# Attention and two FFNs on one core: all softmax sums by way of gathered rows, weights of V with 65 columns and full last key tiles, first head and first layer in another order

## The chip, the cores and the metric

The kernel runs on one core of one Trainium2 chip. The metric is the device time of one execution in microseconds (us). TensorE does the matrix products, VectorE (DVE) and ScalarE (ACT) the elementwise work, GpSimd (POOL) a few fills and the DMA issues of the sums, SyncE (SP) all other DMA issues.

## What is computed

Four batches (B = 4), eight heads (H = 8) of 576 positions (S) and head size 64 (D). First attention with a causal mask and a bias from running sums, then two FFNs:

```python
scores = q @ k^T / 8
cum = cumsum(max(s, 0));  bias = min(-(cum[query] - cum[key]), 0)
attn = exp(masked(scores + bias) - max);  attn /= sum(attn) + 1e-9
x = heads side by side of (attn @ v)                      # (B, 576, 512)

h = max(x @ w_in, 0)                                      # 512 -> 1024
c = three-tap convolution of h over the positions
x1 = (h * sigmoid(c)) @ w_out                             # 1024 -> 512

u = x1 + (V^T U^T applied over the positions of x1)       # rank 32
out = u + max(u @ w_ch1, 0) @ w_ch2                       # 512 -> 2048 -> 512
```

## The kernel before

Each tensor of the FFN is held transposed (channels on partitions, 576 positions in the free dimension, in halves of 288), split into a high and a low part, so that each product is three matmuls (function `three`).

**Attention** of one head runs in five steps, g = 0 to 4. The queries are 576 columns and the keys come in five tiles of 128 rows; the last one starts at 448, so that its first 64 rows repeat keys of tile 3, and only its last 64 are used. First the maximum of each query is found. `max_scores` makes scores with queries on partitions in three rounds (`ROUNDS`), `maxima` on VectorE reduces them, `max_transpose` turns the maxima into a row on TensorE and `max_to_row` on ScalarE writes it as row 96 of `qc`. This is done one head ahead. Then `scores` makes scores with keys on partitions in four chunks, `exponentials` takes exp of each on ScalarE, and `values` multiplies with V, chunk c in step g = c + 1; these are float32 matmuls, two instructions for each product. In the text a "visit" is one such call. The tile `va` held V in 64 of its 128 columns and ones in the other 64, in the order of the head's parity, so that the sums of the exponentials come out on 64 partitions beside the 64 of the result. `evict_head` copies both out of PSUM. The tile of the last keys was used from its row 64 on (`lo = tile_rows(t)[0]`).

Head h + 2 is prepared during head h: ScalarE writes `kb` and `qb` (rounded), VectorE their low parts (`key_low`, `query_low`). In batch 0 VectorE also copies the high parts (`highs`); from head 10 on ScalarE does that.

**Normalising.** For pairs 0 to 2 of a batch's four pairs of heads, one row of sums per head goes by `gather_sums` (DMA) onto 64 partitions of 9 numbers each, is inverted there (`invert_few`), stored (`store_few`), and read back broadcast to all partitions (`spread_few`, two DMAs); `normalise_few` multiplies. For pair 3 `evict_head` copied the 64 rows of sums, and `normalise` did two reciprocals of 128x288 and two products. Then `x_high` (ScalarE) and `x_low` (VectorE) split the pair, which is a fourth of the first layer's contraction; the pairs of a batch must all be there for its first item, `wi`.

**Order.** Each engine executes lists written out by hand. Batch 0's attention runs alone (`ATT_STEPS`, 40 steps). Then batch a's attention is run beside the FFN of batch a - 1, whose items (`wi`, `gated`, `wo`, `turn`, `rank`, `mix`, `up`, `down`, each for a half) `spread` deals to the steps by estimated costs; for a = 1 the first three steps stay empty. What is left after the last attention is the list `END`. An item's PSUM bank is reused two items later (in `END` four). `attention_step` is called before the items of a step and `then` behind them. VectorE runs its `then(a, h, g)`, and in batch 0 after it the low half of a block of weights at g = 2 of the heads in `WEIGHTS_HEADS`, and at `UV_AT` the splitting of U and V. All engines take their instructions in order.

```python
for (h, g), beside in zip(ATT_STEPS, PLAN[a]):
    attention_step(a, h, g)
    for item in beside:
        ffn_step(item)
    if then:
        then(a, h, g)
```

## Time and profile before

| | |
|---|---|
| median of 3 runs (lowest to highest) | 934.64 us (931.06 to 935.13) |
| the profiled execution's own time | 932.81 us |
| its span in the trace | 931.0 us |
| TensorE matmuls busy | 883.0 us (95%), 6184 instructions |
| VectorE busy | 482.5 us (52%), 992 |
| ScalarE busy | 373.2 us (40%), 709 |
| GpSimd busy | 40.4 us (4%), 83 |
| mean granted TensorE clock | 0.987 |

In the rows below "start us, us" are the start and the duration of the first to the last of the merged instructions; "[2.39 <-DVE x_hl L877]" says that the engine sat idle 2.39 us before it, until that instruction. Matmuls are pipelined: their durations overlap, so the pace is read from the distances of their starts. A float32 product with its high and low part counts as two instructions. PEclk is the granted clock as a share of 2.4 GHz.

### The profile page before, as it was taken

How to read it: one execution, taken by the hardware profiler on the slowest of the kernel's cores; microseconds unless marked ns; L12 is line 12 of the kernel's file. 1: busy time of each engine (PE TensorE's matmuls, PEld its weight loads, DVE VectorE, ACT ScalarE, POOL GpSimd, SP SyncE). 2: the span in 40 equal slices, each digit the busy share in tenths (PEclk: the TensorE clock that was granted, in tenths of full speed). 3: DMA queues.
4: the chain of work that ended last, by engine and by line, in shares of the span. 5: the costliest groups of instructions: out<-in, count | busy, mean ns of one | idle time of the engine just before them, and what ended most of it. 6: DMA issues, size and time to landing. Idle time of an engine off the chain costs nothing.

```text
span 931.0 us, 15627 instructions
## 1 busy us (share of the span) xinstructions
PE 883.0 (95%) x6184; PEld 833.6 (90%) x6184; DVE 482.5 (52%) x992; ACT 373.2 (40%) x709; POOL 40.4 (4%) x83
## 2 busy tenths in 40 slices
PE   3988898989999999999999999999999999999998
PEld 2766798969999999898999999988999999999998
DVE  6677796364447852645335872356324670442222
ACT  2656585464334644534323653344221441321110
POOL 3011000010000000000000000001000000000000
PEclk9989999999999999999999999999999999999999
DMA  6576455643764546546444433534343434454441
GB/s 169 125 193 177 126 168 182 232 125 99 242 219 147 171 139 181 202 113 198 153 152 156 168 148 126 167 123 143 116 149 136 180 138 161 157 187 169 150 180 51
DMA packets 63340, 147.04 MB, mean 158 GB/s; under 512 B 29482, under 2 KB 43818, under 8 KB 50980
## 3 DMA queue, kind: packets, MB, share of 16 engines
q1 hardware_dynamic: 60964, 142.40, 46.8%
q0 software_dynamic: 2304, 3.65, 1.5%
q8 instruction: 49, 0.80, 0.4%
q14 instruction: 23, 0.19, 0.1%
HBM read 115.87 MB, written 30.09 MB: 157 GB/s over the span
## 4 chain that ended last, share of the span: by engine, by line
PE 81%; DVE 10%; ACT 5%; issue 3%; DMA 1%; SPq 0%; POOL 0%; ACTq 0%; DVEq 0%
PE psum L1143 22%; PE psum L1145 21%; PE psum L1144 21%; PE psum L1124 8%; PE psum L1071 3%; PE psum L1103 2%; PE psum L1101 2%; DVE psum L849 2%; DVE kb L828 1%; PE psum L1108 1%; DVE qb L836 1%; DVE sums L869 1%; DVE work L914 1%; ACT qc L650 1%; ACT kb L635 1%
## 5 line engine op out<-in xcount | busy, mean ns | idle before, releaser
L1143 PE MATMUL psum<-uu_hl,ring 128*128 128x288 f32 x512 | 155.7, 304 | 7.4 <-DVE uu_hl L952 2.8
L1143 PE MATMUL psum<-r_hl,ring 128*128 128x288 f32 x512 | 154.4, 302 | 1.1 <-DVE u_acc L969 1.1
L1145 PE MATMUL psum<-uu_hl,ring 128*128 128x288 f32 x512 | 151.5, 296 | 0.0
L1144 PE MATMUL psum<-uu_hl,ring 128*128 128x288 f32 x512 | 151.4, 296 | 0.0
L1145 PE MATMUL psum<-r_hl,ring 128*128 128x288 f32 x512 | 151.2, 295 | 0.0
L1144 PE MATMUL psum<-r_hl,ring 128*128 128x288 f32 x512 | 151.1, 295 | 0.0
L1124 PE MATMUL psum<-probs,va 128*128 128x320 f32 (+4 forms) x448 | 124.1, 391 | 6.4 <-ACT probs L656 6.4
L957 DVE SCALAR_TENSOR_TENSOR r_hl<-psum,r_hl 128x288 fp32r<-128x288 f32 x128 | 58.4, 457 | 132.6 <-ACT r_hl L748 132.6
L748 ACT ACTIVATE r_hl<-psum 128x288 fp32r<-128x288 f32 x128 | 52.4, 410 | 181.3 <-PE psum L1145 181.2
L849 DVE CUSTOM_DVE_ANT_0 psum<-psum,key_late 128x512 f32<-128x512 f32 (+4 forms) x160 | 84.8, 564 | 60.3 <-PE psum L1071 59.8
L656 ACT ACTIVATE probs<-psum 128x320 f32<-128x320 f32 (+2 forms) x128 | 61.4, 501 | 115.2 <-PE psum L1108 86.8
L1143 PEld LDWEIGHTS psum<-uu_hl,ring 128*128 128x128 f32 x512 | 96.8, 189 | 11.2 <-DVE uu_hl L952 4.4
L1143 PEld LDWEIGHTS psum<-r_hl,ring 128*128 128x128 f32 x512 | 96.6, 189 | 3.7 <-DVE u_acc L969 1.8
L1144 PEld LDWEIGHTS psum<-uu_hl,ring 128*128 128x128 f32 x512 | 96.9, 189 | 0.3
L1144 PEld LDWEIGHTS psum<-r_hl,ring 128*128 128x128 f32 x512 | 96.6, 189 | 0.6
L1145 PEld LDWEIGHTS psum<-uu_hl,ring 128*128 128x128 f32 x512 | 96.7, 189 | 0.0
L1145 PEld LDWEIGHTS psum<-r_hl,ring 128*128 128x128 f32 x512 | 96.5, 188 | 0.0
L969 DVE TENSOR_TENSOR u_acc<-psum,u_acc 128x288 f32<-128x288 f32 x96 | 43.2, 456 | 102.2 <-PE psum L1145 102.2
L1124 PEld LDWEIGHTS psum<-probs,va 128*128 128x128 f32 (+1 forms) x448 | 75.9, 196 | 16.4 <-ACT probs L656 8.7
L1143 PE MATMUL psum<-x_hl,ring 128*128 128x288 f32 x256 | 79.3, 310 | 4.0 <-DVE x_hl L877 3.4
L1101 PE MATMUL psum<-qb,kb 128*128 128x320 f32 (+4 forms) x224 | 80.8, 378 | 2.1 <-ACT qc L650 1.2
L1143 PE MATMUL psum<-ybuf,ring 128*128 128x288 f32 x256 | 76.7, 300 | 0.0
(103 smaller groups left out, 1648.1 us busy)
## 6 DMA issues: line engine op xcount, KB each, us to landing
ring<-w_scratch SPq DMA_DIRECT2D x72, 1024.0 KB, 4.8
w_scratch<-ring SPq DMA_DIRECT2D x24, 1024.0 KB, 5.3
kq_raw<-in_kq_t SPq DMA_DIRECT2D x64, 288.0 KB, 5.2
stage<-in_w_ch SPq DMA_DIRECT2D x16, 512.0 KB, 5.2
out_t<-u_acc SPq DMA_DIRECT2D x16, 288.0 KB, 4.0
va<-in_v SPq DMA_DIRECT2D x32, 128.0 KB, 2.3
spread_out<-few_scratch POOLq DMA_DIRECT2D x24, 144.0 KB, 3.5
stage<-in_w_in SPq DMA_DIRECT2D x4, 512.0 KB, 7.5
```

Of the source, the lines that this page charges most:

```text
L656: act.activation(probs[:, c % 2, 0:WIDTH[c]], psum[:, c % 2, 0:WIDTH[c]], ACT.Exp).then_inc(exps.sem, 1)
L748: act.activation(r_hl[0][:, f, cols(half)], half_at("up", b, unit, f, half), ACT.Relu).then_inc(rh.sem, 1)
L849: dve.tensor_tensor_reduce(psf[:, at:at + width], psf[:, at:at + width], key_late[:, S - width:S], 1.0, LEAST, ALU.add, ALU.max, row_max[: ...
L957: dve.scalar_tensor_tensor(out=r_hl[1][:, f, cols(half)], in0=half_at("up", b, unit, f, half), scalar=0.0, in1=r_hl[0][:, f, cols(half)].b ...
L969: dve.tensor_tensor(u_acc[:, d, cols(half)], half_at("down", b, unit, d, half), so_far[:, d, cols(half)], ALU.add)\
L1071: mm = pe.matmul(psf[:, at + j:at + e], qc[i][0:CROWS, q0:q0 + P], kc[n % KCS][0:CROWS, j:e], start=bank not in started, stop=True, skip_g ...
L1101: pe.matmul(o, kb[i][:, k0:k0 + P], qb[i][:, i0:i1], start=(x == 0), stop=False, skip_group_check=True)
L1103: mm = pe.matmul(o, kc[n % KCS][:, k0:k0 + P], qc[i][:, i0:i1], start=False, stop=True, skip_group_check=True)
L1124: mm = pe.matmul(psf[:, O0 + i0:O0 + i1], va[i][lo:P, t, :], probs[lo:P, c % 2, at:at + w], start=first, stop=True, skip_group_check=True)
L1143: pe.matmul(o, hi, m_hi, start=start, stop=False)
L1144: pe.matmul(o, hi, m_lo, start=False, stop=False)
L1145: return pe.matmul(o, lo, m_hi, start=False, stop=stop)
```

## The change

- `va` holds V in columns 0 to 63 and ones in column 64 for both parities. `values` uses 65 columns as weights and writes partitions 0 to 64. The first 64 rows of the last key tile are zeroed once, and the product runs over all 128 rows. So does `rank` over its last tile.
- All four pairs are normalised by gathered sums. `normalise` is gone. Pair 3 is inverted and normalised in the next batch's head 0: at steps (0, 1) and (0, 4) beside batch 1, at (0, 0) and (0, 1) beside batches 2 and 3, and in `END` before items 2 and 5. A gather now waits for the copy of the sums alone.
- Beside batch 1 six steps stay empty of FFN items. Pair 2 of batch 0 is normalised at head 7, pairs 0 and 1 one step sooner within heads 4 and 6 (g = 2). The low parts of pairs 0 and 1 move from g = 0 to g = 2. Pairs 2 and 3 are split at steps (0, 0) and (1, 0) of batch 1.
- First head: VectorE does head 0's low parts and maxima before it copies head 1; the last round of scores has PSUM banks of its own, and needs no wait. For all other heads that round's wait is split by bank: what goes into the first bank waits for one reduction, the rest for three.
- GpSimd starts its fills for heads 1 and 2 after the running sums; TensorE waits for the last fill (`s_zero`) only before the first attention step.
- The fourth block of weights is prepared at head 5 for head 6, U and V are split at (3, 2) for (3, 4).

```diff
@@ -239,10 +238,14 @@
+        def max_at(n, r, t):
+            return MAX_AT[t][0] - 2 * BANK * (n == 0 and r == 2), MAX_AT[t][1]
         GROUPS = 5
-        WEIGHTS_HEADS = [1, 2, 4, 6]
-        UV_AT = (3, 4)
+        WEIGHTS_HEADS = [1, 2, 4, 5]
+        UV_AT = (3, 2)
@@ -326,10 +329,9 @@
                   for a in range(1, B)}
-        PLAN = {a: spread(BESIDE[a], len(ATT_STEPS) - 3 * (a == 1), 3 * (a == 1), a == 1) for a in BESIDE}
+        PLAN = {a: spread(BESIDE[a], len(ATT_STEPS) - 6 * (a == 1), 6 * (a == 1), a == 1) for a in BESIDE}
         END = order(B - 1, second(B - 2, UNITS // 2, UNITS)) + flat(second(B - 1, 0, UNITS))
-        END_NORMALISE = (0, 1)
-        END_SPLIT = 2
+        END_INVERT, END_NORMALISE, END_SPLIT = 2, 5, 6
@@ -411,7 +413,11 @@
         X_SPLIT = [{(5, 0): 0, (7, 0): 1}, {(3, 4): 0, (5, 4): 1, (7, 4): 2}]
-        X_SPLIT_LAST = [{}, {(0, 2): (NPAIR - 2, NPAIR - 1)}, {(0, 2): (NPAIR - 1,)}]
+        X_SPLIT_LAST = [{}, {(0, 0): (NPAIR - 2,), (1, 0): (NPAIR - 1,)}, {(0, 2): (NPAIR - 1,)}]
+        NORMALISE = [(4, 6, 7), (3, 5, 7)]
+        INVERT_LAST = [(0, 1), (0, 0)]
+        NORMALISE_LAST = [(0, 4), (0, 1)]
@@ -444,14 +450,14 @@
                 def load_v(a, h):
-                    n, i, c0 = a * H + h, h % 2, D * (h % 2)
+                    n, i = a * H + h, h % 2
                     if n >= B * H:
                         return
                     mm_pv.wait(sp, n - 2)
                     of = v[source(a, h)]
-                    sp.dma_start(va[i][:, 0:NT - 1, c0:c0 + D],
+                    sp.dma_start(va[i][:, 0:NT - 1, 0:D],
                                  of[0:(NT - 1) * P, :].rearrange("(t p) d -> p t d", p=P)).then_inc(v_in[i].sem, 16)
-                    sp.dma_start(va[i][P - D:P, NT - 1, c0:c0 + D], of[(NT - 1) * P:S, :]).then_inc(v_in[i].sem, 16)
+                    sp.dma_start(va[i][P - D:P, NT - 1, 0:D], of[(NT - 1) * P:S, :]).then_inc(v_in[i].sem, 16)
@@ -574,6 +580,8 @@
                 pool.wait_ge(s_mask, 6)
+                pool.wait_ge(s_scan, 1)
@@ -585,30 +593,35 @@
                 copied.wait(pool, 0)
                 for i in range(2):
-                    pool.memset(va[i][:, :, D * (1 - i):D * (1 - i) + D], 1.0)
+                    pool.memset(va[i][:, :, D:D + 1], 1.0).then_inc(s_va, 1)
+                pool.wait_ge(s_va, 2)
+                for i in range(2):
+                    pool.memset(va[i][0:P - D, NT - 1, 0:D + 1], 0.0).then_inc(s_va, 1)
+                pool.wait_ge(s_va, 4)
                 pool.memset(uv_stage[:, :, :], 0.0).then_inc(s_zero, 1)
                 def gather_sums(a, h):
                     x = h % 2
-                    pool.wait_ge(evict.sem, evict.value(a * H + h))
+                    pool.wait_ge(evict.sem, evict.value(a * H + h, 1))
                     row = sums[D * (1 - x):D * (1 - x) + 1, h // 2 % 2, :]
                     pool.dma_start(few[0][x * D:(x + 1) * D, :], row).then_inc(few_in.sem, 16)
                 def store_few(a, pair):
-                    pool.wait_ge(few_done.sem, few_done.value(a * (NPAIR - 1) + pair))
+                    pool.wait_ge(few_done.sem, few_done.value(a * NPAIR + pair))
                     pool.dma_start(few_scratch[a * NPAIR + pair].rearrange("x (p c) -> (x p) c", p=D), few[1][:, :])\
                         .then_inc(few_out.sem, 16)
                 def spread_few(a, pair):
-                    pool.wait_ge(few_out.sem, few_out.value(a * (NPAIR - 1) + pair))
+                    pool.wait_ge(few_out.sem, few_out.value(a * NPAIR + pair))
                     pool.wait_ge(norm.sem, norm.value(a * NPAIR + pair - 1))
...
                 for a in range(B):
-                    for pair in range(NPAIR - 1):
+                    for pair in range(NPAIR):
@@ -660,18 +673,12 @@
-                    if h // 2 == 1:
-                        norm.wait(act, m - 2)
-                    elif m >= 2:
-                        few_in.wait(act, (m - 2) // NPAIR * (NPAIR - 1) + (m - 2) % NPAIR)
-                    if h // 2 < NPAIR - 1:
-                        act.activation(sums[sm:sm + 1, h // 2 % 2, :], psf[sm:sm + 1, O0:O0 + S], ACT.Identity, bias=EPS)\
-                           .then_inc(evict.sem, 1)
-                    else:
-                        act.activation(sums[o:o + D, h // 2 % 2, :], psf[sm:sm + D, O0:O0 + S], ACT.Identity, bias=EPS)\
-                           .then_inc(evict.sem, 1)
+                    if m >= 2:
+                        few_in.wait(act, m - 2)
+                    act.activation(sums[sm:sm + 1, h // 2 % 2, :], psf[D:D + 1, O0:O0 + S], ACT.Identity, bias=EPS)\
+                       .then_inc(evict.sem, 1)
                     xl_done.wait(act, m - NPAIR)
-                    act.activation(x_raw[o:o + D, h // 2, :], psf[o:o + D, O0:O0 + S], ACT.Copy).then_inc(evict.sem, 1)
+                    act.activation(x_raw[o:o + D, h // 2, :], psf[0:D, O0:O0 + S], ACT.Copy).then_inc(evict.sem, 1)
@@ -845,12 +852,12 @@
                     for t in ROUNDS[r]:
-                        at, width = MAX_AT[t]
+                        at, width = max_at(n, r, t)
                         dve.tensor_tensor_reduce(psf[:, at:at + width], psf[:, at:at + width], key_late[:, S - width:S], 1.0, LEAST,
                                                  ALU.add, ALU.max, row_max[:, t:t + 1]).then_inc(red.sem, 1)
                 def invert_few(a, pair):
-                    m = a * (NPAIR - 1) + pair
+                    m = a * NPAIR + pair
@@ -859,18 +866,8 @@
                     evict.wait(dve, a * H + 2 * pair + 1)
-                    dve.wait_ge(spread_in.sem, spread_in.value(a * (NPAIR - 1) + pair))
+                    dve.wait_ge(spread_in.sem, spread_in.value(a * NPAIR + pair))
                     dve.tensor_tensor(x, x, spread_out[:, :], ALU.mult).then_inc(norm.sem, 1)
-                def normalise(a, pair, half):
-                    x, total = x_raw[:, pair, cols(half)], sums[:, pair % 2, cols(half)]
-                    evict.wait(dve, a * H + 2 * pair + 1)
-                    dve.reciprocal(total, total).then_inc(recip.sem, 1)
-                    recip.wait(dve, a, half + 1)
-                    mul = dve.tensor_tensor(x, x, total, ALU.mult)
-                    if half:
-                        mul.then_inc(norm.sem, 1)
@@ -880,28 +877,30 @@
                         maxima(a, h + 1, r)
-                    if (h, g) in X_SPLIT[a > 0]:
-                        x_low(a, X_SPLIT[a > 0][h, g])
+                    if a and (h, g) in X_SPLIT[1]:
+                        x_low(a, X_SPLIT[1][h, g])
                     for pair in X_SPLIT_LAST[min(a, 2)].get((h, g), ()):
                         x_low(a - 1, pair)
                 def then(a, h, g):
+                    if not a and g == 2 and (h, 0) in X_SPLIT[0]:
+                        x_low(a, X_SPLIT[0][h, 0])
                     if g == 3 and not a:
...
                         invert_few(a, h // 2 - 1)
-                    if g == 3 and h in ((3, 5, 7) if a else (4, 6)):
-                        normalise_few(a, (h - 1) // 2 - 1)
+                    if g == 2 + (a > 0) and h in NORMALISE[a > 0]:
+                        normalise_few(a, NORMALISE[a > 0].index(h))
                     if g == 2 and a:
                         key_low(a, h + 2)
                     if g == 3 and a:
                         query_low(a, h + 2)
-                    if (a, h, g) == (1, 0, 1):
-                        normalise_few(0, NPAIR - 2)
-                    if g <= 1 and h == 0 and a:
-                        normalise(a - 1, NPAIR - 1, g)
+                    if a and (h, g) == INVERT_LAST[a > 1]:
+                        invert_few(a - 1, NPAIR - 1)
+                    if a and (h, g) == NORMALISE_LAST[a > 1]:
+                        normalise_few(a - 1, NPAIR - 1)
@@ -1005,11 +1004,11 @@
                 highs(0, 0)
-                highs(0, 1)
                 key_low(0, 0)
                 query_low(0, 0)
                 for r in range(len(ROUNDS)):
                     maxima(0, 0, r)
+                highs(0, 1)
@@ -1030,8 +1029,10 @@
                 for x, item in enumerate(END):
-                    if x in END_NORMALISE:
-                        normalise(B - 1, NPAIR - 1, END_NORMALISE.index(x))
+                    if x == END_INVERT:
+                        invert_few(B - 1, NPAIR - 1)
+                    if x == END_NORMALISE:
+                        normalise_few(B - 1, NPAIR - 1)
@@ -1043,7 +1044,6 @@
                 pe.wait_ge(s_mask, 6)
-                pe.wait_ge(s_zero, 1)
@@ -1058,16 +1058,16 @@
                         mrow.wait(pe, n - 1)
-                    if r == 2:
-                        red.wait(pe, n, 3)
                     started = set()
                     for t in ROUNDS[r]:
-                        at, width = MAX_AT[t]
+                        at, width = max_at(n, r, t)
                         q0 = tile_start(t)
...
                             e = min(width, (bank + 1) * BANK - at)
+                            if r == 2 and n and bank not in started:
+                                red.wait(pe, n, 1 if bank == MX // BANK else 3)
@@ -1118,10 +1118,10 @@
                     for t, i0, i1 in reversed(CHUNKS[c]):
-                        lo, w = tile_rows(t)[0], i1 - i0
+                        w = i1 - i0
                         at -= w
                         first = (c, t) in ((0, 1), (3, 0))
-                        mm = pe.matmul(psf[:, O0 + i0:O0 + i1], va[i][lo:P, t, :], probs[lo:P, c % 2, at:at + w],
+                        mm = pe.matmul(psf[0:D + 1, O0 + i0:O0 + i1], va[i][:, t, 0:D + 1], probs[:, c % 2, at:at + w],
@@ -1203,9 +1203,8 @@
                     for t in range(NT):
-                        lo = tile_rows(t)[0]
-                        u = [x[lo:P, t, :] for x in u_hl]
-                        m = [x[lo:P, t, half * w:(half + 1) * w] for x in x1t_hl]
+                        u = [x[:, t, :] for x in u_hl]
+                        m = [x[:, t, half * w:(half + 1) * w] for x in x1t_hl]
@@ -1251,6 +1250,7 @@
                 max_transpose(0, 0)
+                pe.wait_ge(s_zero, 1)
```

## Rows read from the trace of the kernel before

**Rows 1.** Windows: length, busy (count) of PE, PEld, DVE, ACT, POOL, clock, DMA.

```profile
60.00:65.00 5.00, 5.00 (x20) 4.03 (x19) 2.40 (x6) 2.00 (x4) 0.00 (x0) 0.50 0.46 97
...
200.00:250.00 50.00, 46.09 (x308) 42.48 (x307) 27.42 (x60) 23.39 (x41) 2.12 (x4) 0.93 0.49 148
...
750.00:800.00 50.00, 50.00 (x382) 50.00 (x381) 17.67 (x30) 13.19 (x28) 0.00 (x0) 1.00 0.46 169
```

**Rows 2.** Timeline of the first head's maxima.

```profile
10.27 1.19 PE L1071 MATMUL psum<-kc,qc 66*128 66x512 f32 x3 [10.27 <-DVE kc L819]
...
12.24 0.70 DVE L849 CUSTOM_DVE_ANT_0 psum<-psum,key_late 128x512 f32<-128x512 f32 x1
...
14.99 0.43 DVE L849 CUSTOM_DVE_ANT_0 psum<-psum,key_late 128x256 f32<-128x256 f32 x1 [1.16 <-PE psum L1071]
...
16.93 0.64 ACT L650 ACTIVATE qc<-psum 1x576 fp32r<-1x576 f32 x1 [6.65 <-PE psum L1084]
```

**Rows 3.** Timeline of one period of batch 0's attention.

```profile
42.95 0.64 ACT L650 ACTIVATE qc<-psum 1x576 fp32r<-1x576 f32 x1
...
48.51 0.64 PE L1071 MATMUL psum<-kc,qc 66*128 66x256 f32 x3 [0.55 <-DVE row_max L849]
...
51.14 0.64 ACT L650 ACTIVATE qc<-psum 1x576 fp32r<-1x576 f32 x1
...
52.52 0.45 DVE L819 CAST kc<-kb 64x576 fp32r<-64x576 f32 x1 [2.12 <-ACT kb L635]
```

**Rows 4.** Timeline around U and V, and their last load's time to landing (first 60 us).

```profile
48.82 0.58 SPq L473 DMA_DIRECT2D x_raw<-in_V  x1
...
x_raw<-in_V SPq DMA_DIRECT2D x3, 72.0 KB, 3.2
...
55.03 0.49 DVE L1023 CAST u_hl<-hid 128x640 fp32r<-128x640 f32 x1
...
59.20 1.06 PE L1071 MATMUL psum<-kc,qc 66*128 66x256 f32 x3 [3.05 <-DVE row_max L849]
...
63.51 0.64 ACT L650 ACTIVATE qc<-psum 1x576 fp32r<-1x576 f32 x1
```

**Rows 5.** Timeline of the gathered sums in batch 0; the last row: time to landing (88 to 97 us).

```profile
67.53 0.70 DVE L863 TENSOR_TENSOR x_raw<-x_raw,spread_out 128x576 f32<-128x576 f32 x1
...
84.39 0.22 DVE L857 RECIPROCAL few<-few 128x9 f32<-128x9 f32 x1
...
88.83 1.04 POOL L608 DMA_DIRECT2D spread_out<-few_scratch  x2 [3.35 <-DMA few_scratch<-few]
...
spread_out<-few_scratch POOLq DMA_DIRECT2D x2, 144.0 KB, 2.9
```

**Rows 6.** The sums' tile (min/median/max ns, first to last start), then TensorE where the FFN begins.

```profile
L869 DVE RECIPROCAL sums<-sums x8: 1941/1942/1948, 93.9 to 718.5; 128x288 f32<-128x288 f32 x8
...
101.92 0.40 PE L1143 MATMUL psum<-x_hl,ring 128*128 128x288 f32 x1 [2.39 <-DVE x_hl L877]
...
107.67 0.40 PE L1143 MATMUL psum<-x_hl,ring 128*128 128x288 f32 x1
```

**Rows 7.** TensorE's timeline: third and fourth visit of a head beside the FFN.

```profile
354.84 1.02 PE L1124 MATMUL psum<-probs,va 128*128 128x192 f32 x4
...
355.84 0.30 PE L1144 MATMUL psum<-ybuf,ring 128*128 128x288 f32 x1
...
358.90 0.43 PE L1084 MATMUL psum<-ident_r,row_max 128*1 128x128 f32 x5
359.18 1.26 PE L1124 MATMUL psum<-probs,va 128*128 128x256 f32 x6
...
360.60 0.30 PE L1144 MATMUL psum<-ybuf,ring 128*128 128x288 f32 x1
```

**Rows 8.** TensorE's timeline: rank products, first instruction on 64 rows.

```profile
192.17 0.28 PE L1145 MATMUL psum<-ybuf,u_hl 128*128 128x256 f32 x1
192.38 0.38 PE L1143 MATMUL psum<-ybuf,u_hl 64*128 64x256 f32 x1
192.60 0.27 PE L1144 MATMUL psum<-ybuf,u_hl 64*128 64x256 f32 x1
```

3 lines of the change are left out of this document (1 added, 2 removed).

## The prediction

> **What bounds the kernel now.** I read the page first: TensorE is busy 95% of the span, VectorE 52%, ScalarE 40%. Then the busy time by windows, which splits the run in two. In a late window 382 matmuls start in 50 us, one per 0.131 us, with no idle [rows 1]. There only less TensorE work helps. The waits by window put TensorE's idle time elsewhere: at the start, in batch 0's attention, and where the first layer of the FFN begins. So I read the timeline there, engine by engine, and last the timeline of the V products and of the rank products where TensorE is saturated.
>
> Batch 0's attention is a ring, not a TensorE bound. ScalarE writes the row of maxima at 42.95 and the next at 51.14, a period of 8.19 us. Inside it VectorE does copies, low parts and maxima, then TensorE gets the last round of scores at 48.51 after 0.55 us of idle, and VectorE sits idle 2.12 us before the next copies at 52.52, 1.4 us behind the row of maxima [rows 3]. Work put on VectorE ahead of 52.52 is free up to 2.1 us. Work put after it lengthens the period one for one.
>
> **The change part by part.**
>
> *Full last key tile.* Of the V products of one head, the pieces of the third visit (192 and 320 columns, two instructions each) start at 354.84. The second matmul behind them starts at 355.84. Less one pace of 0.131 that is 0.87 us for 512 columns, 1.70 ns a column. The fourth visit (256, 128 and 64 columns) runs from 359.18 to 360.60, less 0.131 is 1.29 us, where 448 columns by that rate are 0.76 [rows 7]. So 0.53 us is excess, and the only new thing is the piece of 64 rows. The rank products show it alone: from the last 128-row matmul at 192.17 to the second 64-row one at 192.60 is 0.43 us, where two 256-column matmuls take 0.23 [rows 8], so 0.20 for going in. I take as much for coming out. In the V products 0.40 is then the row change and 0.13 the narrow pieces' weight loads. Bounds: 0.40 to 0.53, I take 0.50, as the weights also become narrower. 24 heads lie in the part bound by TensorE, one of them will stand alone after the change: 23 x 0.50 = 11.5 us. In the first 50 us of batch 1's attention VectorE is as full as TensorE, so I take 10.5 (bounds 8 and 12). The rank products: 8 halves x 0.40 = 3.2, I take 3.0.
>
> The Trainium skill (TensorE: Matmul & The Clock Gate, "LDWEIGHTS (loading the stationary operand)") says that a load goes by the weights' columns and that the rows don't matter. By that the full tile is worth nothing, and only the 65 columns give something. The rows on the rank products speak against it.
>
> *First head rearranged.* Before, the maxima of head 0 begin at 12.24 behind the copies of head 1, though TensorE began at 10.27, and VectorE waits 1.16 us again for the second set of scores at 14.99 [rows 2]. Now head 1's copies go behind, and the last round has banks of its own. TensorE's start I leave at 10.27: the running sums' rows come by DMA at about that time, whatever the memsets do (bounds 0 and 0.5). The first maxima can begin near 10.9, so 1.3 + 1.2 = 2.5 us gained, and the first row of maxima comes at 14.4 for 16.93.
>
> *Last round's wait split.* Two of its three matmuls no longer wait for the third reduction. Three take 0.65 us from 48.51 [rows 3], one alone about 0.33. So 0.3 per head in the ring: the period becomes 7.9.
>
> *U and V split two steps sooner.* Today it lies behind the low parts: VectorE at 55.03, TensorE idle 3.05 us until 59.20, the next row of maxima at 63.51, 12.37 us after 51.14 [rows 4]. The granted clock is 0.50 from 60 to 65, the lower level of 1.2 GHz, after that idle [rows 1]. So 4.2 us are lost, 2.5 of VectorE work and 1.7 of clock. Now it comes before the copies, into the 2.1 us hole. But its last load is issued at 48.82 and takes 3.2 [rows 4], landing near 52.0. Relative to the ring that is 1.6 us after VectorE is free at 50.4 (minus 0.1 to 0.5 as the loads start with faster V products). 1.2 to 1.6 of waiting and 2.5 of work, less the hole, leave 1.9 on the ring, and perhaps again a clock drop, for which I add 0.7. Gain 1.6 (bounds 0 and 4.2).
>
> *Normalising of pairs 0 and 1, a step sooner.* 0.70 us each, now in the hole: at 67.53 it delayed the maxima [rows 5]. Gain 0.7 each. Head 6's weight step goes to head 5 to leave room: 1.2 + 0.75 of low part still fit into 2.1. Nothing.
>
> *Normalising of pair 2 in batch 0.* It moves from batch 1 to head 7, step 2. Its chain is long. Inversion at 84.39, spreading issued at 88.83 with the second transfer 0.52 later, 2.9 to land [rows 5]: 7.9 us from inversion to use. VectorE reaches the new place 4 us after the inversion and waits. Behind it queue the copies of head 9, and behind those, on TensorE, the first scores for head 9's maxima and everything after. The rows of maxima now follow at 39.9 (for 42.95: less 2.5 and twice 0.3), 47.8, 58.2 (7.9 + 1.9 + 0.7) and, three periods on, 81.9. The inversion lies behind copies and low parts, by estimate 4 us ahead of the next row of maxima, at 77.9, so the product ends at 86.5 and the copies at 87.4. The copies would have begun at 83.3. TensorE idles some 3 us, and since it fell to the lower clock after 3.05 us once [rows 4], it may again.
>
> *Pair 3 by gathered sums, first layer three steps on.* Off VectorE go eight reciprocals of 1.94 us [rows 6], two per batch, and half products. In come a gather, a tiny reciprocal, a store, two transfers and a product of 0.75. At batch 1's start the inversion follows the second maxima, near 91.1. Then 7.9 to the landing, 0.75 + 0.68 + 0.75 for product, high and low part: TensorE gets the last tile of the first layer at 101.2. The clock may add up to 1.3, and I take 101.8. Before, TensorE resumed the first layer at 101.92 after 2.39 of idle and had the clock back by 107.67 [rows 6]. From 101.92 to 107.67 it did 18 matmuls (2.4 us at the pace of rows 1), the transposes (0.3) and one fourth visit (1.3), 4.0 in all, so 1.75 is lost. To come to the state of the new kernel at 101.8 (three steps of attention, 3.3 us, three matmuls 0.4, the row change 0.4) the old one needs until 101.92 + 4.1 + 1.75 = 107.8. So the lead when the FFN begins is 6.0. For a lower clock there I take off 0.5: 5.5 us. In it the gains above (2.5, 2.1, 1.6, 1.4: 7.6) are mostly kept, and what the reciprocals gave back is eaten by the pair 2 stall. Bounds: 2 (both stalls with a clock drop, the loads late) and 9 (no stall).
>
> At batches 2 and 3 and in the end part steps are over 6 us, so the gather has landed, but the product may wait 1 to 3 us for its transfer. Before, VectorE was held 2.4 us twice at the same place. I count nothing (bounds -1 and +2).
>
> **Sum.** 5.5 + 10.5 + 3.0 = 19.0. The profiled execution took 932.81 (span 931.0), so 913.8; the median of the runs shown is 934.64, 0.2% above. I say 914 us. A change of 0.5% (4.7 us) is about what a measurement can tell.
>
> **Rivals.**
> - *The front does better, 907 us.* If the UV loads land in time and the pair 2 stall is hidden, 3.5 more. Batch 0's FFN meets three fewer steps of attention; from 200 to 250 TensorE idles 3.9 us there and its clock is 0.93 in the mean, 3.5 more [rows 1]. If the new spread misses half of that, 3.7 more. For it: those losses hang on alignment. Against: nothing in the change aims at them. Chance 0.2.
> - *The front gives nothing, 920 us.* Pair 2's and pair 3's transfers come one behind the other and both let the clock fall. For it: the 7.9 us chain is longer than a half head. Chance 0.17.
> - *The row change isn't the cost, 924 us.* Then only the narrow loads shrink, 0.13 us a head, 3.0 in all, and 5.5 come from the front: 932.8 - 8.5 = 924. Against it: rows 8 have no narrow piece. The page's rule above would make it so. Chance 0.06.
> - *Slower: weights of 65 columns cost a column change, 950 us.* If going from 128 columns to 65 and back costs 0.19 each way like the rows, four visits a head give 1.5 us, x24 = 36, so 914 + 36 = 950. It decides from 0.10 us a change. Against it: the transposes of the maxima have weights of one column, five of them start at 358.90 and the next visit at 359.18, 0.28 us for 576 columns, where the rate of rows 1 gives 0.26: no room for such a change [rows 7]. Chance 0.04.
> - The forecast, 909 to 918: 0.53.
>
> Range 904 to 925: it leaves out the slower case and the tails. Faster by over 0.5% (below 930): 0.94. Same 0.02, slower 0.04.
>
> **What would show it.** Right if: the fourth visit takes about 0.8 us and the rank products step evenly over the last tile; the first row of maxima is written near 14.4, the period in batch 0 is 7.9; VectorE waits before the product at head 7, step 2, with TensorE idle about 3 us behind it; the first layer begins near 100; no reciprocal of 288 columns is left. The forecast fails most easily in batch 1, where the new spread meets a full VectorE, and if the clock falls in other places than before.

## The result, and the profile after

| | before | after |
|---|---|---|
| median of 11 runs each (lowest to highest) | 933.73 us (929.55 to 939.12) | 924.72 us (922.69 to 930.27) |
| profiled execution's own time, span | 932.81, 931.0 | 926.22, 924.4 |
| its mean granted TensorE clock | 0.987 | 0.980 |

The ratio is 0.9909, 95% interval 0.9886 to 0.9932: 9.0 us faster where 914 us (19 less) was forecast. It lies in the range, but the change gave less than half of what the sum said.

The engines' totals in the profile of the changed kernel (busy us, share of the span, instructions):

```profile
PE 870.9 (94%) x6184; PEld 816.5 (88%) x6184; DVE 469.0 (51%) x984; ACT 372.3 (40%) x709; POOL 51.5 (6%) x105
```

The rows of maxima are the best milestones, for they come once a head in both kernels. The timeline after, for heads 0, 3, 4, 5, 8 and 16 (start, duration):

```profile
13.88 0.64 ACT L663 ACTIVATE qc<-psum 1x576 fp32r<-1x576 f32 x1 [3.98 <-PE psum L1084]
38.47 0.64 ACT L663 ACTIVATE qc<-psum 1x576 fp32r<-1x576 f32 x1
46.45 0.64 ACT L663 ACTIVATE qc<-psum 1x576 fp32r<-1x576 f32 x1
58.69 0.64 ACT L663 ACTIVATE qc<-psum 1x576 fp32r<-1x576 f32 x1
82.55 0.64 ACT L663 ACTIVATE qc<-psum 1x576 fp32r<-1x576 f32 x1
265.99 0.64 ACT L663 ACTIVATE qc<-psum 1x576 fp32r<-1x576 f32 x1 [5.28 <-PE psum L1084]
```

The same milestones of before are in [rows 2 to 4], and those for heads 8 and 16 are:

```profile
89.34 0.64 ACT L650 ACTIVATE qc<-psum 1x576 fp32r<-1x576 f32 x1
266.87 0.64 ACT L650 ACTIVATE qc<-psum 1x576 fp32r<-1x576 f32 x1 [5.28 <-PE psum L1084]
```

So the lead is 3.05 us at head 0, 4.8 at head 5, 6.8 at head 8, and 0.9 at head 16, which is the start of batch 2. At the end it is 6.6. Nearly the whole front lead, and batch 1's share of the savings with it, is gone between heads 8 and 16.

To see where, I took the windows of 5 us and split every stretch into idle time (length less PE busy), clock loss (PE busy times one less the granted clock) and the rest, TensorE's work at full clock. Each cell is idle + clock loss / work:

| stretch | before | after |
|---|---|---|
| to the row of head 0 | 14.0 + 0 / 2.9 | 11.2 + 0 / 2.6 |
| head 0 to head 8 | 9.6 + 2.7 / 60.1 | 10.2 + 2.8 / 55.7 |
| head 8 to head 16 | 12.0 + 5.4 / 160.1 | 16.4 + 12.0 / 155.0 |
| head 16 to head 31 | 8.5 + 1.5 / 399.9 | 10.7 + 1.6 / 392.1 |
| head 31 to the end | 3.9 + 0 / 250.4 | 4.9 + 0 / 249.1 |

From head 8 on TensorE's work fell by 5.1 + 7.8 + 1.3 = 14.2 us, where 13.5 were forecast. Over the same stretches idle time and clock loss rose from 31.3 to 45.6 us, by 14.3, of which 11.0 lie between heads 8 and 16. The saving was real, and the schedule paid it back behind head 8.

These are single executions, and a milestone of one carries 1 to 2 us of chance. The old order's program is the same up to head 8 in before, e8, e12 and e15 but for e8's full tile, and still its first period (row of head 0 to row of head 1) took 9.64, 9.65, 8.84 and 7.89 us. The shown execution of the changed kernel also took 1.5 us more than its median. In e10 below, which differs by one empty step and whose profiled execution took 924.37 us, the lead is 6.8 us at head 8 and 4.7 at head 16, with 17.4 + 6.5 lost between them. So the direction is safe, but of the 11.0 us a few belong to this execution.

The first part of the loss behind head 8 is the stall for pair 2. VectorE's, GpSimd's and TensorE's timeline after, in order of the chain (the last two rows are pair 3's inversion and the first layer's beginning):

```profile
78.47 0.21 DVE L864 RECIPROCAL few<-few 128x9 f32<-128x9 f32 x1
83.77 1.04 POOL L621 DMA_DIRECT2D spread_out<-few_scratch  x2 [4.21 <-DMA few_scratch<-few]
88.50 0.76 DVE L870 TENSOR_TENSOR x_raw<-x_raw,spread_out 128x576 f32<-128x576 f32 x1 [6.07 <-DMA spread_out<-few_scratch]
90.09 0.77 PE L1071 MATMUL psum<-kc,qc 66*128 66x512 f32 x1 [5.41 <-issue]
94.26 0.21 DVE L864 RECIPROCAL few<-few 128x9 f32<-128x9 f32 x1
103.27 0.34 PE L1143 MATMUL psum<-x_hl,ring 128*128 128x288 f32 x1
```

From the inversion to the product it is 10.0 us, for the 7.9 taken from [rows 5]. VectorE waits 6.07 us and TensorE 5.41. The windows after (columns as in [rows 1]) show TensorE standing, then half the clock, and once more behind waits from 198 to 206 us, the longest of them 1.66 us in the mix stage:

```profile
85.00:90.00 5.00, 0.00 (x0) 0.00 (x0) 1.50 (x4) 2.23 (x5) 0.84 (x2) 0.92 0.95 298
90.00:95.00 5.00, 4.91 (x16) 3.71 (x17) 3.80 (x10) 0.60 (x1) 0.23 (x1) 0.50 0.45 114
95.00:100.00 5.00, 5.00 (x24) 3.67 (x23) 2.57 (x6) 3.47 (x6) 1.37 (x3) 0.55 0.23 66
200.00:205.00 5.00, 2.39 (x15) 1.60 (x14) 3.33 (x7) 3.50 (x7) 0.52 (x1) 1.00 0.45 113
205.00:210.00 5.00, 4.36 (x14) 3.18 (x14) 3.64 (x11) 2.53 (x5) 0.00 (x0) 0.53 0.15 35
210.00:215.00 5.00, 5.00 (x19) 4.14 (x18) 2.42 (x8) 2.54 (x5) 0.00 (x0) 0.50 0.01 4
```

A clock of 0.50 is the lower level, 1.2 GHz. The stall for pair 2 is new. The one near 205 us is not, for before has it too, somewhat shorter:

```profile
200.00:205.00 5.00, 3.32 (x20) 2.34 (x19) 4.70 (x11) 4.69 (x8) 0.00 (x0) 1.00 0.12 28
205.00:210.00 5.00, 3.50 (x14) 2.44 (x13) 3.13 (x7) 2.78 (x5) 0.52 (x1) 0.55 0.49 121
210.00:215.00 5.00, 4.77 (x26) 4.10 (x25) 3.23 (x11) 2.97 (x5) 0.00 (x0) 0.76 0.09 14
```

### The profile page after: what moved, and what is told of

Its sections match the earlier page's. It is cut to its first block, busy times and chain, and to the rows that moved or that the text cites. A ratio compares the mean times of both kernels' runs of the same rounds, so it can differ in the third digit from the quotient of the medians.

```text
span 924.4 us, 15651 instructions
## 1 busy us (share of the span) xinstructions
PE 870.9 (94%) x6184; PEld 816.5 (88%) x6184; DVE 469.0 (51%) x984; ACT 372.3 (40%) x709; POOL 51.5 (6%) x105
## 4 chain that ended last, share of the span: by engine, by line
PE 74%; DVE 9%; issue 8%; ACT 5%; DMA 3%; POOL 0%; DVEq 0%; ACTq 0%; POOLq 0%
PE psum L1143 20%; PE psum L1145 19%; PE psum L1144 19%; PE psum L1124 7%; PE psum L1071 3%; PE psum L1103 2%; PE psum L1101 2%; DVE psum L856 2%; DMA spread_out<-few_scratch 1%; DMA few_scratch<-few 1%; ACT qc L663 1%; DVE work L913 1%; PE psum L1108 1%; DVE work L916 1%; DVE kb L835 1%
## 5 line engine op out<-in xcount | busy, mean ns | idle before, releaser
L1124 PE MATMUL psum<-probs,va 128*65 128x320 f32 (+4 forms) x448 | 114.4, 376 | 4.1 <-ACT probs L669 4.1
L1143 PEld LDWEIGHTS psum<-uu_hl,ring 128*128 128x128 f32 x512 | 97.0, 189 | 11.2 <-DVE u_acc L968 4.4
L1143 PE MATMUL psum<-ybuf,ring 128*128 128x288 f32 x256 | 77.5, 303 | 2.2 <-DVE ybuf L928 2.2
L1145 PE MATMUL psum<-ybuf,ring 128*128 128x288 f32 x256 | 76.1, 297 | 0.0
```

The source lines that it names most:

```text
L1124: mm = pe.matmul(psf[0:D + 1, O0 + i0:O0 + i1], va[i][:, t, 0:D + 1], probs[:, c % 2, at:at + w], start=first, stop=True, skip_group_check ...
L1143: pe.matmul(o, hi, m_hi, start=start, stop=False)
L1145: return pe.matmul(o, lo, m_hi, start=False, stop=stop)
```

## The experiments

Times are medians, each measured beside the kernel before, whose median stood at 933.4 to 933.7 us. The ratio is to that kernel. The diffs show the main lines of each edit, and lines are shortened by "...". Edits are against the changed kernel unless it says otherwise.

### Which part of the weights' change is worth what

**Rows of the last tile (e1).**

```diff
-                        mm = pe.matmul(psf[0:D + 1, ...], va[i][:, t, 0:D + 1], probs[:, c % 2, at:at + w],
+                        mm = pe.matmul(psf[0:D + 1, ...], va[i][lo:P, t, 0:D + 1], probs[lo:P, c % 2, at:at + w],
```

> The changed kernel with the V products of the last key tile over its last 64 rows again (65 columns stay; rank stays full). Theory (the row change costs 0.20 us each way, TensorE bound in 23 heads): the fourth visit takes 0.4 us more, 8 to 10 us in all, so 933 us, about the kernel before. Rival (much of TensorE's saving is given back where VectorE or ScalarE sets the pace beside batch 0's FFN): 14 to 16 heads count, 929 to 931. Second rival (only the narrow weight loads count): within 1 us of the changed kernel, 925.

925.78 us, ratio 0.9922 (0.9899 to 0.9945): 1.1 us above the changed kernel, far under what the visits' size asks for (below). By its time alone this is the second rival's number, but the visit itself speaks against that rival.

**Columns (e2).** The weights get their 128 columns back, all ones beyond V.

```diff
-  psf[0:D + 1, O0 + i0:O0 + i1], va[i][:, t, 0:D + 1]
+  psf[:, O0 + i0:O0 + i1], va[i][:, t, :]
```

> The changed kernel with V's weights 128 columns wide again, 63 more columns of ones, full last tile kept. Theory: the narrow pieces' weight loads cost about 0.05 to 0.1 us a head, 925.5 to 927. Rival (the columns carry the gain of the fourth visit): 0.4 us a head, 931 to 934.

929.87 us, ratio 0.9952 (0.9933 to 0.9971): 5.2 us above, between the two forecasts. The fourth visit, with the next matmul behind it, in the timelines of the changed kernel, e1 and e2:

```profile
358.01 0.95 PE L1124 MATMUL psum<-probs,va 128*65 128x256 f32 x6
358.99 0.29 PE L1144 MATMUL psum<-ybuf,ring 128*128 128x288 f32 x1
```

```profile
355.87 1.10 PE L1124 MATMUL psum<-probs,va 128*65 128x256 f32 x6
357.13 0.30 PE L1144 MATMUL psum<-ybuf,ring 128*128 128x288 f32 x1
```

```profile
358.65 1.07 PE L1124 MATMUL psum<-probs,va 128*128 128x256 f32 x6
359.75 0.29 PE L1144 MATMUL psum<-ybuf,ring 128*128 128x288 f32 x1
```

Less one pace of 0.131, as in the prediction, the visit takes 0.85 us in the changed kernel, 1.13 with 64 rows, 0.97 with 128 columns, and 1.29 before [rows 7]. So the full tile is worth 0.28 to 0.32 us a head, the narrow weights 0.12 to 0.16, both 0.44 (forecast 0.50). By the visits e1 should have cost 23 x 0.28 = 6.4 us and e2 2.8 to 3.7; they cost 1.1 and 5.2. Kept in the same books, their traces have 862.0 and 858.2 us of TensorE's work, where the changed kernel has 854.5: 7.5 and 3.7 more, about what the visits say. What moved otherwise is idle time and clock loss, 62.2 us in e1 and 70.0 in e2 for 69.9. A visit's size says what TensorE's work is, and the time moved otherwise by up to 5 us.

**Full tile alone, in the old order (e8).** Against the kernel before:

```diff
-                        mm = pe.matmul(psf[:, ...], va[i][lo:P, t, :], probs[lo:P, c % 2, at:at + w],
+                        mm = pe.matmul(psf[:, ...], va[i][:, t, :], probs[:, c % 2, at:at + w],
...
-                        u = [x[lo:P, t, :] for x in u_hl]
+                        u = [x[:, t, :] for x in u_hl]
```

> The kernel before with full last key tiles alone, in the V products and the rank products: weights stay 128 columns wide, all schedules and the sums as before. By the fourth visits measured so far it takes 0.3 us a head (24 beside the FFN) and 3.1 us in the rank products off TensorE, 10.5 us. Theory (what TensorE saves counts in full): 923 to 924. Rival (beside batch 0's FFN it counts for nothing: 16 heads and 6 halves of rank products, 7 us): 926 to 927.5. Second rival (the row change isn't the cost): 932 to 934.

927.78 us, ratio 0.9935 (0.9914 to 0.9957): 5.9 us gained, though 23 x 0.30 + 3.2 = 10.1 less work was to be done. The theory's 923 to 924 is missed.

### The order by itself

**Order alone (e9).** 128 columns and the 64 rows are put back in the V products, and the 64 rows in `rank`: the edits of e1 and e2 together, and e8's edit of `rank` reversed.

> The changed kernel with the old matmuls: weights of V with 128 columns, and the last key tile by its last 64 rows in the V products and in the rank products. What is left of the change is the order: first head, pairs normalised sooner, pair 3 by gathered sums, first layer three steps on. If the two halves of the change add up, this gives what the old order with full tiles did not: 933.7 - 9.0 + 5.9 = 930.6, 3 us below the kernel before. By the prediction's sum the order is worth 5.5 us, so 928. If the order's lead is lost by batch 1 whatever the matmuls are, 933 to 934. If the savings overlap (both lose the same 4 us in batch 1), 927 or less.

932.56 us, ratio 0.9993 (0.9975 to 1.001). The order that I had priced at 5.5 us gives 1.1, not told from nothing. Timelines of e9, rows of maxima 8 and 16:

```profile
83.95 0.64 ACT L663 ACTIVATE qc<-psum 1x576 fp32r<-1x576 f32 x1
266.44 0.64 ACT L663 ACTIVATE qc<-psum 1x576 fp32r<-1x576 f32 x1 [5.28 <-PE psum L1084]
```

The lead is 5.4 us at head 8 and 0.4 at head 16. So the loss is the order's own, and needs neither the new weights nor the full tile.

**Old order, first layer three steps later (e15).** Against the kernel before, one number:

```diff
-        PLAN = {a: spread(BESIDE[a], len(ATT_STEPS) - 3 * (a == 1), 3 * (a == 1), a == 1) for a in BESIDE}
+        PLAN = {a: spread(BESIDE[a], len(ATT_STEPS) - 6 * (a == 1), 6 * (a == 1), a == 1) for a in BESIDE}
```

> The kernel before with six empty steps in place of three at the start of batch 1's attention, nothing else changed. Its wait for pair 3 when the first layer resumes (2.39 us, and 1.4 of lower clock behind it) lies then beside attention. Theory A: the fewer the steps that are left for batch 0's FFN, the more of its chains' waits stay uncovered (130 to 160 and 180 to 220 us), so what the later start gives is lost again: 932 to 936. Theory B, the wait for pair 3 is simply saved and the density is free: 929 to 930.

936.64 us, ratio 1.0046 (1.0026 to 1.0066): 3.1 us slower. Moving the first layer three steps on costs time even in the old kernel, where it takes away the wait of 2.39 us [rows 6]. Timelines of e15, VectorE, then TensorE:

```profile
96.62 1.94 DVE L869 RECIPROCAL sums<-sums 128x288 f32<-128x288 f32 x1
98.60 0.46 DVE L871 TENSOR_TENSOR x_raw<-x_raw,sums 128x288 f32<-128x288 f32 x1
99.32 0.80 DVE L849 CUSTOM_DVE_ANT_0 psum<-psum,key_late 128x576 f32<-128x576 f32 x1
100.23 0.43 PE L1084 MATMUL psum<-ident_r,row_max 128*1 128x128 f32 x5 [2.56 <-DVE row_max L849]
```

And its windows there:

```profile
95.00:100.00 5.00, 2.33 (x14) 1.55 (x12) 4.97 (x11) 2.13 (x4) 0.00 (x0) 1.00 0.66 166
100.00:105.00 5.00, 4.45 (x18) 3.59 (x19) 2.87 (x6) 4.72 (x9) 0.52 (x1) 0.55 0.13 29
```

VectorE is full in these attention steps, TensorE has only attention, so it runs dry and the clock goes to the lower level. The first layer had been the work that filled such waits. Between heads 8 and 16 the old order loses 12.0 + 5.4 us and e15 13.9 + 11.1 (idle + clock), 7.6 more for the same work (160.1, 159.8). Up to the first layer's last quarter with three more steps of attention done it is 5.6 for before (to 107.8, the prediction's estimate of that state) and 7.9 for e15 (to 108.7), and from there to head 16 12.3 and 16.7. So most of it comes later, where batch 0's FFN is dealt into 34 steps in place of 37. That the denser steps leave the same chains less to cover them is my reading. (One execution each; e15's had won 1.9 us by chance before head 3, and before lost 1.5 us more than e15 behind head 16.)

e15 and e9 have the same number of empty steps and the same matmuls, and reach the first layer in the same state: at 107.46 and 102.92 us, 4.5 apart. Their medians are 936.64 and 932.56, 4.1 apart. So the order without the later first layer is worth about 4.1 us (2 to 7 by the two intervals), it is kept to the end, and the later first layer takes 3.1 of it back. That gives e9's 1.1. Three empty steps in the new order were not run, so that the new order too pays these 3.1 us is argued.

### Was it a full VectorE?

**One tap (e7), two taps (e14).** In batch 0 the third tap of the convolution is done on 8 of 576 columns, in e14 (and e12, e13) the first as well; most of these taps is left out.

```diff
-                    dve.scalar_tensor_tensor(out=conv[i], in0=hid[:, i, 2:S + 2], ...
+                    w = S if b else 8
+                    dve.scalar_tensor_tensor(out=conv[i][:, 0:w], in0=hid[:, i, 2:w + 2], ...
```

> The changed kernel with the convolution's third tap of batch 0 done on 8 of 576 columns, so that it leaves out most of that tap: eight VectorE instructions of 0.82 us become 0.1. TensorE's work is the same. Theory (VectorE, 4.9 of 5 us busy from 113 to 153, sets the pace there and takes TensorE's saving): the two idle times of TensorE of 1.8 and 2.2 us in that stretch and the clock drops behind them shrink, 919 to 921.5. Rival (TensorE sets the pace, the losses are the steps' alignment): 924 to 925.5.

923.37 us, ratio 0.9883 (0.9856 to 0.9909): 1.4 us under the changed kernel, between the two forecasts and within the noise.

> The changed kernel with the same two taps cut. Cutting one of them gave 1.3 us. Theory: the lead at the end of batch 1's attention grows from 1 to 5 or more, 918 to 920. Rival: as with the one tap, 922 to 923, because the loss in that stage is TensorE's waits for single chains and its clock, not VectorE's sum.

921.35 us, ratio 0.9883 (0.9862 to 0.9903): 3.4 us under the changed kernel, again between the two. (A ratio near that of e7, though the median is 2 us lower, shows the size of the noise.) In its trace the lead at head 16 is 5.7 us, as the theory said, but it is 4.7 in e10 without any cut.

**The same two taps in the old order (e12) and in the order alone (e13).**

> The kernel before, with two of the three taps of batch 0's convolution done on 8 of 576 columns (most of these two taps is left out). That takes 8 x 2 x 0.74 = 11.8 us off VectorE between the first layer and the end of batch 1's attention, and nothing off TensorE. By itself it says how much the old kernel lost to a full VectorE there: theory 2 to 5 us (928 to 932), as TensorE idles 2.7 us at 140 to 150 and falls to the lower level once. Rival: nothing (933.5 within 1).

930.59 us, ratio 0.9971 (0.9955 to 0.9987).

> The changed order with the old matmuls (128 columns, 64 rows of the last key tile in V and rank products), with the same two taps cut. Theory: the order's lead of 5.5 us is there when the first layer begins and is eaten where VectorE is full beside batch 1; with VectorE relieved 3 to 5 us of it survive, so this comes out 3 to 5 us under the old order with cut taps (924 to 928). Rival: the lead is lost in other places (the empty steps squeeze the FFN's items, the clock), and the difference stays near 1 us as without the cut.

932.48 us, ratio 0.9992 (0.9976 to 1.0008). With 11.8 us of VectorE work gone the new order is 1.9 us behind the old one instead of 1.1 ahead. The same cut is worth 2.8 us in the old kernel, 3.4 in the changed one and 0.1 in the order alone (932.56 in e9). So a full VectorE beside batch 0's FFN costs something in two of three kernels, but it is not what eats the order's lead. That theory falls.

### Moving the waits

**Pair 2 later (e3).** It is normalised at (0, 1) of batch 1 again and split at (0, 2), and head 7's entry in `NORMALISE` goes.

```diff
+                    if (a, h, g) == (1, 0, 1):
+                        normalise_few(0, NPAIR - 2)
```

> The changed kernel with pair 2 of batch 0 normalised at head 0, step 1 of batch 1 instead of head 7, step 2, and split at step 2 instead of 0. Theory (the 5.4 us of idle and the lower clock behind that product are lost for good): the stall goes, the first layer begins 3 to 5 us sooner, 920 to 921.5. Rival (a lead at the start of batch 1 is given back in waits of its FFN, whose chains VectorE and ScalarE set): 924 to 925.

925.16 us, ratio 0.992 (0.9892 to 0.9947): no gain, the rival's number. Timelines of e3, VectorE, then TensorE:

```profile
91.67 0.22 DVE L864 RECIPROCAL few<-few 128x9 f32<-128x9 f32 x1 [0.42 <-DMA few<-sums]
100.24 0.76 DVE L870 TENSOR_TENSOR x_raw<-x_raw,spread_out 128x576 f32<-128x576 f32 x1 [4.91 <-DMA spread_out<-few_scratch]
102.57 0.40 PE L1145 MATMUL psum<-x_hl,ring 128*128 128x288 f32 x1 [2.80 <-DVE x_hl L874]
```

Pair 2's stall is gone, and pair 3's chain of 8.6 us is the next wait, with TensorE idle 2.80 us.

**Pair 3 later as well (e5).** e3's edit, and pair 3 normalised at (1, 1) and split at (1, 2), with eight empty steps.

```diff
-        X_SPLIT_LAST = [{}, {(0, 0): (NPAIR - 2,), (1, 0): (NPAIR - 1,)}, {(0, 2): (NPAIR - 1,)}]
+        X_SPLIT_LAST = [{}, {(0, 2): (NPAIR - 2,), (1, 2): (NPAIR - 1,)}, {(0, 2): (NPAIR - 1,)}]
-        NORMALISE_LAST = [(0, 4), (0, 1)]
+        NORMALISE_LAST = [(1, 1), (0, 1)]
```

> The changed kernel with pair 2 as in the experiment before, and pair 3 of batch 0 normalised at step (1, 1) and split at (1, 2) of batch 1, first layer begun at the eighth step. Theory (pair 2's and pair 3's transfers are what TensorE waits for, one behind the other, and the clock falls behind either): no idle of TensorE over 1 us between 84 and 105 us and no window there under clock 1.00. The first layer begins about 3 us later than with pair 2 moved alone, yet three steps of attention further on; end 919 to 921.5. Rival (VectorE sets the pace beside the first layer, and what is won ahead of it is given back): 923.5 to 925.5.

921.54 us, ratio 0.987 (0.9844 to 0.9896): 3.2 us under the changed kernel. What the theory asked of the trace is there: between 84 and 105 us TensorE's longest idle time is 0.99 us, and every window of 5 us has clock 1.00.

**Only the number of empty steps, five (e10) and eight (e11).**

```diff
-        PLAN = {a: spread(BESIDE[a], len(ATT_STEPS) - 6 * (a == 1), 6 * (a == 1), a == 1) for a in BESIDE}
+        PLAN = {a: spread(BESIDE[a], len(ATT_STEPS) - 8 * (a == 1), 8 * (a == 1), a == 1) for a in BESIDE}
```

> The changed kernel with five empty steps in place of six at the start of batch 1's attention, so that the first layer begins one step sooner; no work is added or taken away. Theory: the first layer's last quarter then waits for pair 3 about one step (1.1 us) longer, and the FFN's steps fall elsewhere on the VectorE-bound stretch: 922 to 928, and TensorE's work (span less idle less clock) stays at 854 within 1 us while idle plus clock loss moves. Rival: the placement is neutral, and the time stays at 924.7 within 1 us, with the loss at 70 us.

925.18 us, ratio 0.9906 (0.9891 to 0.9921): as the changed kernel. TensorE's work in the trace is 853.7 us, so only the losses moved.

> The changed kernel with eight empty steps in place of six: the first layer begins two steps later, when pair 3 has long landed, and its items are squeezed into 32 steps. Theory: pair 2's stall stays (it lies ahead of the steps), so the gain of the version with both transfers moved is not to be had by the empty steps alone: 924 to 927. Rival: the later first layer alone made the gain of 3 us there: 921 to 922. TensorE's work stays at 854 within 1 us.

926.65 us, ratio 0.9924 (0.9904 to 0.9943). That is 1.9 us above the changed kernel, which the intervals don't tell from nothing; the work is 854.4. So e5's gain isn't from its eight steps. It is from the two waits: against e11, e5 is 5.1 us better.

**Loads of U and V sooner (e4).** The three `load_small` calls go to steps (0, 3), (0, 4) and (1, 3).

```diff
-                    if g == 4 and h < 3:
-                        load_small(h)
+                    if (h, g) in ((0, 3), (0, 4), (1, 3)):
+                        load_small(((0, 3), (0, 4), (1, 3)).index((h, g)))
```

> The changed kernel with the small loads of U and V issued at steps (0, 3), (0, 4), (1, 3) instead of (0, 4), (1, 4), (2, 4), so that they have landed when VectorE splits U and V. Theory: VectorE's wait of 1.35 us for the load and the overrun of the ring shrink, and with them TensorE's idle of 2.9 us and the lower clock up to 59 us: 3 to 4 us earlier there, 921 to 922 at the end. Rival (given back in batch 1): the row of maxima at 58.7 comes 3 us sooner but the end within 1 us, 924 to 925.

921.33 us, ratio 0.9871 (0.984 to 0.9902): 3.4 us under the changed kernel, as the theory said, though its six executions spread from 918.11 to 928.13. In the trace the rows of maxima 4 and 5 are 8.97 us apart (46.73 and 55.70) in place of 12.24.

**All three (e6): e5 and e4 together.**

> The kernel above with the small loads of U and V sooner as well. Theory: the gains add, 3.4 for the loads to that of the kernel above: 915.5 to 918. Rival (given back): 921 to 922, no better than the early loads alone.

919.61 us (919.0 to 920.25), ratio 0.985 (0.9825 to 0.9875), the fastest of all. The single gains of 3.2 and 3.4 give 5.1 together, so they add in part, and the time lies between the forecasts. Its rows of maxima 8 and 16 come at 78.50 and 253.58, the lead at head 16 is 13.3 us. Windows of e6 in the place of the stall:

```profile
85.00:90.00 5.00, 3.12 (x23) 2.23 (x23) 3.54 (x9) 4.58 (x8) 0.76 (x2) 1.00 0.58 169
90.00:95.00 5.00, 4.65 (x31) 3.56 (x30) 1.86 (x7) 2.54 (x6) 1.36 (x3) 1.00 0.79 203
```

The clock stays full, with 54 matmuls where the changed kernel did 16 in the same two windows.

**The same order with the old matmuls (e16).** e6's edits on e9.

> The new order with the old matmuls, and with the three edits of the best version so far (pair 2 and pair 3 normalised later, loads of U and V sooner, eight empty steps). In the full kernel these were worth 5.1 us (924.7 to 919.6). If they stand by themselves, 932.6 - 5.1 = 927.5, and the order is then worth 6 us of the 14 and the matmuls 8. If they only paid through the faster matmuls, 931 to 933.

927.31 us, ratio 0.9936 (0.9915 to 0.9957). Against e9 it is 5.3 us better, as e6 against the changed kernel (5.1). The worth of moving the waits doesn't depend on the matmuls. It also shows that the order, with its waits moved, is worth 6.3 us (933.56 less 927.31), even with eight empty steps.

## Why the prediction was right in sign and over twice too large

**The step that failed** is the term of 5.5 us, "lead when the FFN begins". I compared the two kernels at one equal state, the first layer's last quarter, 101.8 against 107.8. In the trace the first layer begins at 103.27 and its last quarter at 104.51, so the lead there was 3.3 us in place of 6.0. e9 against e15, which have their empty steps in common, puts the front at 4.1 us of time. The larger miss lies behind that state, where I took all as equal, so that dealing batch 0's FFN into 34 steps in place of 37 stood in the sum at nothing. e15 measured this with nothing else changed, in the old order: 3.1 us slower (interval 2.4 to 6.2 from the ratio). 4.1 less 3.1 is about what e9 measured for the whole term, 1.1 us (interval -1 to 2). The prediction had named the new spread as the place where the forecast fails most easily, and the three fewer steps and the idle time from 200 to 250 us as a rival by which it might go better, but gave its sum no cost for them.

**A saving of TensorE's work counted in full.** The terms 10.5 and 3.0 were right as work: from e9 to the changed kernel the work from head 8 on falls by 3.7 + 7.7 + 1.5 = 12.9 us (e9's is 158.7, 399.8, 250.6). In time the pair differs by 7.8 (932.56 less 924.72), and in the old order 10.1 gave 5.9. So this term failed too: the work was right, and its worth in time was counted in full where 7.8 of 12.9 us came. The sum priced matmuls where TensorE is busy, not where TensorE next waits for a chain: there, a faster TensorE only arrives sooner. From e9 to the changed kernel idle time and clock loss rise from 23.8 to 28.4 us between heads 8 and 16, and from 14.2 to 17.2 from there to the end.

So 19.0 = 5.5 + 13.5 became 8.9 = 1.1 + 7.8. This split is shown by e9. That the 7.8 falls short through waits is read from the accounting, not shown for each wait.

**Point by point.**

- First head: 16.93 to 13.88, 3.05 us for 2.5. TensorE began at 9.66 for 10.27, so its start did move, by 0.6, a little past my bound of 0.5.
- Period in batch 0: 46.45 less 38.47 is 7.98 for 7.9. Right.
- U and V: from row 4 to row 5 12.24 us, before 12.37 [rows 4]. A gain of 1.6 was forecast, and 0.1 came. VectorE waited 1.35 us for the load, within the 1.2 to 1.6 forecast, and began at 47.06. But the first copy behind the splitting took 1.40 us in place of 0.45, and TensorE idled 2.94. e4, which takes the loads' wait away, brings row 5 to 55.70. The term was mis-sized by 1.5 us, within its bounds, and the slow copy, which it did not have, is about 1 us of that (last section).
- Pair 2: the place and the kind were right, the size not: 5.4 us idle for 3, and behind it most of 10 us at the lower level, a loss of 4.91 x 0.50 + 5.00 x 0.45 = 4.7. The clock loss of this stretch was taken as 0.5. The chain of 7.9 us was one reading of a time that varies: the transfers from and to the scratch store took 1.7 to 7.5 us to land in before's trace.
- Full tile and narrow weights: 0.44 a head for 0.50. The rank products step evenly:

```profile
192.25 0.28 PE L1144 MATMUL psum<-ybuf,u_hl 128*128 128x256 f32 x1
192.37 0.28 PE L1145 MATMUL psum<-ybuf,u_hl 128*128 128x256 f32 x1
192.49 0.70 PE L1124 MATMUL psum<-probs,va 128*65 128x320 f32 x2
```

  From 192.25 on each is 0.12 apart, where [rows 8] had 0.43 for two. So the rival that the row change isn't the cost is out: e1 alone puts 0.28 back. The Trainium skill (TensorE: Matmul & The Clock Gate, "LDWEIGHTS (loading the stationary operand)") says that the rows of a weight load don't matter. It speaks of the load, and for that before's trace agrees: the loads of `rank`, with 64 rows and with 128, all take 0.18 to 0.19 us. The measured cost sits where the rows change from 128 to 64 and back.
- The rival of slower column changes is out too: the visit with 65 columns is the shortest.
- The rival "the front gives nothing", 920 us, was near in part of its reason: pair 2's transfer stalls and the clock falls, and e3 shows pair 3's wait behind it. But the denser FFN was not in it, and its time was too low, as it counted the matmuls' 13.5 in full.

**What stays open.** e1, e2 and e8 move the time by 1 to 5 us away from their visits' sum. The dealing of items to steps decides which chain meets which wait, and I have no experiment that prices each wait between 130 and 220 us. How e15's 3.1 us divides between the dry steps ahead of the first layer and the denser dealing is read from one execution each. Whether fewer empty steps would keep more of the new order's lead isn't settled either, as pair 3 lands too late for three of them and only five, six and eight were run.

## What to carry to other kernels

- Work that is moved off a stretch in which another engine is full was that stretch's filling. Price the stretch that it leaves (idle time and lower clock) and the denser one that it enters, not only the wait that it takes away. One run with only that number changed shows it (e15). To price the rest of a change, compare two kernels that share that number (e9 with e15).
- After a saving, keep the books by milestones: idle, clock loss and work for each stretch. Here the work fell as computed to within 1 us, and the whole error stood in the other two columns. Read the milestones of more than one execution, for each carries 1 to 2 us of chance.
- Two waits in a row hide each other. Removing the first alone gave nothing (e3), the second as well gave 3.2 us (e5): follow each chain from its inversion to its use and give both the room.

## What the runs showed of the hardware beyond that

- Going from 128 to 64 rows and back costs TensorE about 0.3 us a visit in the V products and 0.4 us a half in the rank products. It is read from the distances of starts; the profile's grouped durations don't point to it. For `rank`, from the start of the last matmul ahead of the last tile to the start of the second matmul behind the product it is 0.99 us in before (809.89 to 810.88) and 0.62 after (803.62 to 804.24).
- A copy of 64x576 on VectorE that takes 0.45 us [rows 3] takes 1.40 us when a fill of 1.07 us begins on GpSimd right behind its start. All thirteen traces in which the two begin together show it (the changed kernel, e1 to e7, e9 to e11, e13 and e14, 1.40 to 1.41). In e16 the fill begins 1.1 us after the copy's end, and the copy takes 0.45; the rows of maxima around it are 7.99 us apart there (45.74, 53.73), where e6, with the same loads and the copy beside the fill, has 8.96 (45.66, 54.62). Not every instruction is held up: in before the same fill runs beside a reduction in PSUM, which takes 0.70 us as in [rows 2]. Timelines of VectorE and GpSimd, first after, then e16:

```profile
49.61 1.40 DVE L826 CAST kc<-kb 64x576 fp32r<-64x576 f32 x1
49.64 1.07 POOL L631 MEMSET hid<- 128x1156 f32 x1 [2.39 <-DVE v L1027]
```

```profile
47.38 0.45 DVE L826 CAST kc<-kb 64x576 fp32r<-64x576 f32 x1
48.93 1.08 POOL L631 MEMSET hid<- 128x1156 f32 x1
```

- The chain from inversion over the scratch store to the broadcast took 7.9 us [rows 5], 8.6 (pair 3 in e3), and in one execution of the changed kernel 10.0 for pair 2 and 6.3 for pair 3 (94.26 to 100.53). A wait that is planned from one reading of it can be off by 2 us.
